# The main expert's two layers as three products of rounded parts, with its raw weights loaded a second time

## The reference

```python
    # attn_out: softmax(q k^T / 8, causal) v, mixed by g with phi(q) M_prev / (phi(q) z_prev)
    x = np.ascontiguousarray(attn_out.transpose(0, 2, 1, 3)).reshape(B * S, H * D)
    # dense part: h = x @ w_in (512 x 2048); g = h, 0 or (h + 1)^2 / 4; x2 = g @ w_out
    logits = x2 @ w_gate
    expert_idx = np.argmax(logits, axis=1)
    # the first 288 tokens of each expert, in order, are kept
    h = np.maximum(np.einsum('ecd,edf->ecf', disp, w1), 0.0)     # 8 x (512 x 1024)
    y = np.einsum('ecf,efd->ecd', h, w2)                         # 8 x (1024 x 512)
    out[i] = gate_w[i] * y[expert_idx[i], pos[i]]                # for kept tokens
```

## Time and profile before

| | |
|---|---|
| median of 3 runs | 315.66 us (315.33 to 315.79) |
| the profiled execution, in all | 316.72 us |
| its span, first to last instruction | 315.0 us |
| mean granted clock of TensorE | 0.999 |
| busy: PE, DVE, ACT, POOL | 307.2, 211.9, 143.5, 122.5 us |

### The profile page before, as it was taken

How to read it: one execution, slowest core, us unless ns; L and a number is a source line. 1 busy time by engine, 2 the same in 40 slices (tenths; PEclk the granted TensorE clock), 3 DMA queues, 4 the chain that set the end, 5 groups by cost and what they waited for, 6 DMA issues and landing times.

```text
span 315.0 us, 6957 instructions
## 1 busy us (share of the span) xinstructions
PE 307.2 (98%) x2697; PEld 249.3 (79%) x2697; DVE 211.9 (67%) x569; ACT 143.5 (46%) x318; POOL 122.5 (39%) x146
## 2 busy tenths in 40 slices
PE   7999999999999999999999999999999999999994
PEld 6566676676677988878999989898989867775764
DVE  4899998999976466987866377657955466612300
ACT  1777865866965144555633353335343322101020
POOL 4777997998998200735860030003000000100121
PEclk9999999999999999999999999999999999999999
DMA  8999986861456600000002229530042075099720
GB/s 158 172 203 213 228 210 104 201 182 34 139 141 143 205 0 2 2 0 2 0 2 37 40 67 401 132 51 1 2 75 40 0 301 235 12 370 402 293 76 10
DMA packets 75047, 38.48 MB, mean 122 GB/s; under 512 B 66008, under 2 KB 66016, under 8 KB 73988
## 3 DMA queue, kind: packets, MB, share of 16 engines
q1 hardware_dynamic: 72340, 36.74, 44.6%
q10 hardware_dynamic: 2416, 0.59, 1.0%
q0 software_dynamic: 256, 0.67, 0.7%
HBM read 32.66 MB, written 5.39 MB: 121 GB/s over the span
## 4 chain that ended last, share of the span: by engine, by line
PE 94%; DVE 3%; issue 1%; POOL 1%; POOLq 0%; DVEq 0%
PE bank_a L1725 17%; PE bank_b L1725 16%; PE bank_out L1682 6%; PE bank_b L1785 4%; PE bank_pt L1785 4%; PE bank_a L1583 4%; PE bank_pt L1635 4%; PE bank_a L1659 3%; PE bank_b L1937 3%; PE bank_a L1937 3%; PE bank_b L1946 3%; PE bank_a L1946 3%; PE bank_b L1578 2%; PE bank_out L1758 2%; PE bank_out L1679 2%; PE bank_out L2074 2%
## 5 line engine op out<-in xcount | busy, mean ns | idle before, releaser
L687 POOL TENSOR_SCALAR prob<-prob,rl,gate_loc 128x512 f32<-128x512 f32 (+3 forms) x64 | 41.7, 665 | 11.8 <-DVE rl L1144 11.8
L1725 PE MATMUL bank_a<-x_hi,win_hi 128*128 128x288 f32 x128 | 39.3, 307 | 0.0
L1725 PE MATMUL bank_b<-x_hi,win_hi 128*128 128x288 f32 x128 | 38.1, 297 | 0.0
L1725 PE MATMUL bank_b<-x_lo,win_hi 128*128 128x288 f32 x128 | 38.0, 297 | 0.0
L1725 PE MATMUL bank_a<-x_lo,win_hi 128*128 128x288 f32 x128 | 38.0, 297 | 0.0
L1725 PE MATMUL bank_b<-x_hi,win_lo 128*128 128x288 f32 x128 | 38.0, 297 | 0.0
L1725 PE MATMUL bank_a<-x_hi,win_lo 128*128 128x288 f32 x128 | 38.0, 297 | 0.0
L923 ACT ACTIVATE g_raw<-bank_a,biases 128x576 f32<-128x576 f32 x16 | 11.9, 743 | 53.3 <-DVE sq L1221 53.3
L860 ACT ACTIVATE prob<-prob,negmax 128x512 f32<-128x512 f32 (+3 forms) x64 | 35.0, 549 | 0.8 <-DVE negmax L1094 0.8
L716 POOL TENSOR_TENSOR x_lo<-xT,x_hi 128x1152 fp32r<-128x1152 f32 x4 | 10.6, 2662 | 63.5 <-ACT x_hi L873 63.5
L1227 DVE TENSOR_TENSOR g_raw<-g_raw,sq 128x576 f32<-128x576 f32 x32 | 31.3, 979 | 0.5 <-ACT sq L924 0.5
(11 more groups left out here) (309 smaller groups left out, 746.6 us busy)
## 6 DMA issues: line engine op xcount, KB each, us to landing
w_sb<-in_moe_w_dram SPq DMA_DIRECT2D x6, 2048.0 KB, 13.9
win_raw<-in_moe_w_in_dram SPq DMA_DIRECT2D x4, 1024.0 KB, 5.8
wout<-in_moe_w_out_dram SPq DMA_DIRECT2D x4, 1024.0 KB, 5.8
win_raw<-in_moe_w_in_dram SPq DMA_DIRECT2D x1, 4096.0 KB, 13.5
out_dram<-zero_row SPq DMA_DIRECT2D x8, 288.0 KB
x_d<-x_rows SPq DMA_DIRECT2D x32, 72.0 KB, 2.1
v_sb<-in_v_dram SPq DMA_DIRECT2D x16, 128.0 KB, 2.6
qn<-in_q_dram SPq DMA_DIRECT2D x24, 72.0 KB, 5.5
```

What stands on the lines that cost most here:

```text
L687: pool.tensor_scalar(prob[u][:, h, :], prob[u][:, h, :], rl[:, c:c + 1], gate_loc[:, 2 * j + h:2 * j + h + 1], ALU.mult, ALU.mult).then_in ...
L1725: last = pe.matmul(h_bank(d)[:, t, :], w[:, m, f:f + P], x[c % 2][:, m, :], start=(m == 0 and n == 0), stop=(m == KT - 1 and n == 2))
```

## The change

- The main expert's layers are made of rounded parts: three products for each fp32 one (`main_first`, `main_second`). `hT` becomes `h_hi` (ACT) and `h_lo` (DVE), `x2T` is split into `x2_hi` (ACT, chunk four, step 5) and `x2_lo` (DVE, chunk four, step 6, before `place`).
- The weights are split while chunks three and four run. ACT rounds w1 in eight blocks (`first_hi`) and w2 in eight (`second_hi`, the last four during the first layer). POOL subtracts the eight of w1 and four of w2, DVE the other four of w2. The lo parts are written over the raw weights in `w1_sb[0]`, `w2_sb[0]`. The hi parts take the places of `xT` and of the x parts.
- Because of that expert 0's raw w1 and w2 are loaded a second time for the left tokens, and the other experts' weights get other places: the first one's is that of `win_hi`, the second one's that of `win_lo`, which is also that of `win_raw`. So w1 of the second waits for `few_hidden` (`s_fh`), and what follows it in SP's list stands behind that wait.
- The second layer runs over f outside and the four outputs inside. `few_x` comes after f = 4, `few_hidden` after f = 5, `few_turned` in the middle of f = 7. `ranks` and `list_tokens` move one tile later.
- The left tokens' experts go in the order 1, 2, 0. Banks are exchanged: the rows' banks become `f_bank[0:3]`, the left tokens' dense part uses `bank_pt` and `bank_o`. `copy_yt` is shared between DVE (0, 1) and ACT (2, 3).

```diff
-        w_at = (w_first_at, xT_at, win_at)
+        w_at = ((w_first_at, w_first_at + 4 * DT * F), (win_at, win_at + 4 * DT * F), (win_lo_at, win_lo_at + 4 * DT * F))
+        w1_hi, _, _ = sb("w1_hi", [P, ET, DM], F32R, at=xT_at)
+        w1_lo, _, _ = sb("w1_lo", [P, DT, F], F32R, at=w_at[0][0])
...
@@ sync
-            expert_weights(0, e0)
+            first_weights(0, e0)
+            second_weights(0, e0)
...
+            sp.wait_ge(s_eh, ET)
+            first_weights(0, e0)
             sp.wait_ge(s_fx, 16)
             sp.wait_ge(s_job, 1)
-            expert_weights(1, sp.value_load(jobs[0:1, 0, 1:2], min_val=0, max_val=E - 1))
-            expert_weights(2, sp.value_load(jobs[0:1, 0, 2:3], min_val=0, max_val=E - 1))
+            others = [sp.value_load(jobs[0:1, 0, k:k + 1], min_val=0, max_val=E - 1) for k in range(1, OTHERS + 1)]
+            first_weights(1, others[0])
+            sp.wait_ge(s_fh, 1)
+            first_weights(2, others[1])
+            second_weights(1, others[0])
+            second_weights(2, others[1])
+            sp.wait_ge(s_ey, DT)
+            second_weights(0, e0)
@@ gpsimd
-            for c in range(2, NCH):
-                x_lo_part(c)
+            x_lo_part(2)
+            for i in range(4):
+                first_lo(i)
+            x_lo_part(3)
+            for i in range(4):
+                second_lo(i)
+            for i in range(4, ET):
+                first_lo(i)
@@ scalar, in chunk(c, first)
+                    if c == 2 and d in (2, 3):
+                        first_hi(2 * d - 4)
+                        first_hi(2 * d - 3)
+                    if c == 3 and d in (0, 1):
+                        second_hi(2 * d)
+                        second_hi(2 * d + 1)
+                    if c == 3 and d in (3, 4):
+                        first_hi(2 * d - 2)
+                        first_hi(2 * d - 1)
+                    if c == 3 and d == 5:
+                        x2_hi_part()
...
+            for f in range(ET):
+                act.wait_ge(s_eh, f + 1)
+                if f == 0:
+                    act.wait_ge(s_g, ND * NCH - 1)
+                act.activation(h_hi[:, f, :], e_bank(f)[:, 0:SLOTS], ACT.Relu).then_inc(s_ehe, 1)
+                if f == 2:
+                    exponentials(NCH)
+                if f in (0, 1, 3, 4):
+                    second_hi((4, 5, 0, 6, 7)[f])
@@ vector
+                    if c == NCH - 1 and d == 6:
+                        x2_lo_part()
                     if c > 0 and d == 6:
                         place(c)
...
             chunks(dve, chunk)
+            hidden_lo(0)
+            hidden_lo(1)
             copy_lt(NCH)
+            hidden_lo(2)
             choose(NCH)
+            second_lo(4)
+            second_lo(5)
+            hidden_lo(3)
             gates_of(NCH)
             place(NCH)
+            hidden_lo(4)
+            hidden_lo(5)
             rank_tokens(NCH)
+            hidden_lo(6)
+            hidden_lo(7)
...
+            second_lo(6)
+            second_lo(7)
             list_jobs()
@@ tensor
+            def main_first(f):
+
+                bank_read(f)
+                pe.wait_ge(s_al, f + 1)
+                if f > 3:
+                    pe.wait_ge(s_ehe, f - 3)
+                    pe.wait_ge(s_hl, f - 3)
+                for m in range(DT):
+                    for n, (w, x) in enumerate(((w1_hi[:, f, m * P:m * P + P], x2_hi), (w1_hi[:, f, m * P:m * P + P], x2_lo),
+                                                (w1_lo[:, m, f * P:f * P + P], x2_hi))):
+                        last = pe.matmul(e_bank(f)[:, 0:SLOTS], w, x[:, m, :], start=(m == 0 and n == 0), stop=(m == DT - 1 and n == 2))
+                last.then_inc(s_eh, 1)
...
+            for f in range(ET):
+                main_first(f)
+                route_between(f)
+            for f in range(ET - 1):
+                main_second(f, range(DT))
+                if f == 4:
                     few_x()
+                if f == 5:
                     few_hidden()
+            main_second(ET - 1, range(2))
+            few_turned()
+            main_second(ET - 1, range(2, DT))
...
-                pe.wait_ge(s_wf[k], 16)
-                pe.wait_ge(s_kte, k + 1)
-                if k == 0:
-                    pe.wait_ge(s_ere, slot_tiles)
+                pe.wait_ge(s_wf[k], 32 if k == 0 else 16)
+                pe.wait_ge(s_kte, ORDER.index(k) + 1)
```

More of the change, by code:

```diff
@@ L241, in build_program @@
         offset[0] = phase
+        y_row = [sb(f"y_row{r}", [ST, DM], F32)[0] for r in range(slot_tiles)]
         x2_few, _, _ = sb("x2_few", [P, DM_PART], F32)
@@ L944, in exponentials, with x2_hi_part, first_hi, second_hi @@
                 act.activation(ex[:, :, :], lg[:, :, :], ACT.Exp).then_inc(s_ex, 1)
+            def x2_hi_part():
+                for n in range(2):
+                    act.wait_ge(s_xst[n], 16 * 4 * NPAIR // 2)
+                act.wait_ge(s_ye, KT)
+                act.activation(x2_hi[:, :, :], x2T[:, :, :], ACT.Copy).then_inc(s_xh, 1)
+            def first_hi(i):
+                if i == 0:
+                    act.wait_ge(s_we[0], 16)
+                    act.wait_ge(s_xre, 4)
+                    act.wait_ge(s_xlo, 2)
+                if i == 4:
+                    act.wait_ge(s_xre, NPAIR)
+                    act.wait_ge(s_xlo, NCH)
+                act.activation(w1_hi[:, i, :].rearrange("p (m c) -> p m c", c=P), w1_sb[0][:, :, i * P:i * P + P], ACT.Copy
+                               ).then_inc(s_ah, 1)
+            def second_hi(i):
+                if i == 0:
+                    act.wait_ge(s_wf[0], 16)
+                    act.wait_ge(s_h, ND * (NCH - 1))
+                if i == 4:
+                    act.wait_ge(s_h, ND * NCH)
+                act.activation(w2_hi[i][:, :], w2_sb[0][:, i, :], ACT.Copy).then_inc(s_bh, 1)
             def chunk(c, first):
@@ L975, in _, with hidden, copy_yt @@
             chunks(act, chunk)
-            def hidden(J, late):
+            def hidden(J):
                 for f in range(ET):
                     act.wait_ge(s_eh, ET * J + f + 1)
-                    if late and f == 0:
-                        act.wait_ge(s_g, ND * NCH - 1)
                     act.activation(hT[:, f, :], e_bank(f)[:, 0:SLOTS], ACT.Relu).then_inc(s_ehe, 1)
-                    if late and f == 2:
-                        exponentials(NCH)
-            hidden(0, True)
+            for f in range(ET):
[7 more added lines that the diff above has]
+                    second_hi((4, 5, 0, 6, 7)[f])
+            def copy_yt(J, m):
+                act.wait_ge(s_ey, DT * J + m + 1)
+                act.activation(yT[:, m, :], e_bank(m)[:, 0:SLOTS], ACT.Copy).then_inc(s_eye, 1)
             act.wait_ge(s_ft, 1)
@@ L1022, in work @@
                     activation_terms(NCH + n, d)
-                hidden(n + 1, False)
+                hidden(n + 1)
             jobs_of(act, work)
@@ L1927, in _, with expert @@
             chunks(pe, chunk)
-            def expert(J, ahead, between, within):
+            def expert(J):
                 for f in range(ET):
-                    ahead(f)
                     if f > 3:
@@ L1947, in expert, with main_second @@
                                          start=(f == 0), stop=(f == ET - 1))
-                        if f == ET - 1:
-                            last.then_inc(s_ey, 1)
-                        within(m, f)
+                    last.then_inc(s_ey, 1)
+            def main_first(f):
[9 more added lines that the diff above has]
+                last.then_inc(s_eh, 1)
+            def main_second(f, outs):
+                pe.wait_ge(s_bl, f + 1)
+                for m in outs:
+                    pe.wait_ge(s_hl, 5 + m if f == 0 else f + 1)
+                    part = slice(m * P, m * P + P)
+                    for n, (w, x) in enumerate(((w2_hi[f][:, part], h_hi), (w2_hi[f][:, part], h_lo), (w2_lo[:, f, part], h_hi))):
+                        last = pe.matmul(e_bank(m)[:, 0:SLOTS], w, x[:, f, :], start=(f == 0 and n == 0), stop=(f == ET - 1 and n == 2))
+                    if f == ET - 1:
+                        last.then_inc(s_ey, 1)
             def expert_rows(J, tiles):
@@ L1998, in few_hidden @@
                 pe.wait_ge(s_fte, 1)
-                pe.wait_ge(s_eye, 1)
+                spread_list()
                 pe.wait_ge(s_win, 16)
@@ L2076, in few_second @@
                                          w2_sb[k][:, f, DM_PART * g:DM_PART * (g + 1)],
-                                         start=(k == 0 and f == 0), stop=(k == OTHERS and f == ET - 1))
-                if k == OTHERS:
+                                         start=(k == ORDER[0] and f == 0), stop=(k == ORDER[-1] and f == ET - 1))
+                if k == ORDER[-1]:
                     last.then_inc(s_ky, 1)
-            for k in range(OTHERS + 1):
+            for k in ORDER:
                 few_first(k)
-            for k in range(OTHERS + 1):
+            for k in ORDER:
```

(4 more changed lines are left out.)

140 lines of the change are left out of this document (84 added, 56 removed).

## The result

| | before | changed |
|---|---|---|
| median | 315.73 us (315.33 to 316.0, 4 runs) | 322.02 us (320.17 to 322.44, 4 runs) |
| the profiled execution, in all | 316.72 us | 322.08 us |
| its span | 315.0 us | 320.3 us |
| mean granted clock of TensorE | 0.999 | 0.987 |

What follows compares the result with a forecast made beforehand. TensorE, 94% of the chain, bounded the kernel. Its 4.2 us gain would become a 4.9 us wait: last landing 309.4 plus 1.8 and 4.4 gives span 315.6, time 316.3 us, range 313.6 to 318.4.

Steps and rivals of the forecast that it cites:

- The products of rounded parts: Main expert's two layers: three products at 0.134 us each replace an fp32 one of 0.51, 6.9 us less TensorE work.
- before `ranks`: End of chunk four: TensorE stands 0.4 us because the new x2_lo delays VectorE's queue.
- before the second logits: End of chunk four: TensorE stands 0.9 us for a later add_terms on VectorE.
- the second layer starts: Main expert's second layer: start at 269.55 against 271.16, a gain of 1.6 of the possible 3.6 us.
- The splits in chunks three and four: Splitting the weights on ScalarE and GpSimd during the hidden layers of these chunks: costed at nothing.
- The gather of x_few and the list of jobs ... are ready before: Ahead of few_hidden: both, made within 5 us of the hot rows, cause no wait; few_hidden ends at 283.6.
- The term of the four loads: Four 2 MB loads issued from 283.7 on, behind few_hidden: 24.2 us plus 1.5 for writes, last landing 309.4.
- The writes of rows: Three writes of finished rows, 0.58 MB, fall amid the four loads: 1.5 us if they queue, 0 if they find gaps.
- C: Last products: TensorE's clock falls while it waits, up to doubling their 1.8 us; time 318.1 us, chance 0.16.
- my own case: End of the kernel: the 4.2 us gain turns into a 4.9 us wait for expert 0's w2; 316.3 us, chance 0.42.
- The base: From span to median: the 0.6 us difference of spans was carried over to the median of 315.66, giving 316.3.
- B: Last products: loads land before TensorE wants them and its 4.2 us gain arrives whole; time 311.5 us, chance 0.12.

Runs made afterwards that it cites:

- e1: The changed kernel without the second load of expert 0's w2, reading the first other expert's w2 instead (output differs): 316.14 us, ratio 1.004.
- e2: The changed kernel without both second loads, expert 0's left products reading the first other expert's weights (output differs): 315.12 us, ratio 1.001.
- e6: The changed kernel with x2_lo made before VectorE's clip of step 6 in chunk four instead of behind it: 320.42 us, ratio 1.0152.
- e8: e7 with x2_lo also made before the clip of step 6 in chunk four: 315.46 us, ratio 1.0002.
- e4: The kernel before with only a second load of the main expert's w1 added, issued 0.7 us after the gather: 315.28 us, ratio 1.0001.
- e3: The changed kernel with w1's second load moved behind the wait for the gather: 320.27 us, ratio 1.0153.
- e5: The changed kernel with 28 unused transposes after each of the first two thirds of the last products: 320.91 us, ratio 1.0181.
- e10: The changed kernel run once more, as it is: 321.22 us, ratio 1.0168.
- e7: The changed kernel without second loads: expert 0 first, from its hi and lo parts, and the first other's w2 loaded before the few_hidden wait: 317.0 us, ratio 1.0047.
- e9: e8 with expert 0's w1 loaded again behind the gather and the first other's w2 back behind few_hidden: 315.29 us, ratio 0.9995.
- e11: e9 with 64 more small instructions at TensorE's start (10 whole and 72 small transposes for 18 whole): 316.69 us, ratio 0.9994.
- e14: e9 with 16 more small instructions at TensorE's start (10 whole and 24 small transposes for 18 whole): 315.77 us, one run.
- e16: e9's program once more, beside e15 on the same chip: 315.31 us, ratio 0.9938.
- e13: The changed kernel with 64 more small instructions at TensorE's start: 323.51 us, ratio 1.02.
- e15: e9 with 56 more small instructions at TensorE's start (4 whole and 70 small transposes for 18 whole): 315.09 us, ratio 0.9939.
- e12: e9 with SyncE's wait for few_hidden moved to the end of the w_out products, keeping queues empty there: 321.31 us, one run.

## Why the prediction came out as it did

**Right, by its own steps.** The products of rounded parts are 0.13 apart, 12 in 1.57 to 1.77 us, as costed. `x2_lo` takes 1.35 us. TensorE stands before `ranks` (0.15 against 0.4) and before the second logits (1.02 against 0.9). The whole trace is some 0.4 us late, already at the load of w1 at 186.26 (185.87 before), ahead of every new instruction of the change; the traces of the other runs that start like it have this load at 185.4 to 186.5, so it is scatter. Apart from that the second layer starts at 269.7 (270.06 - 0.4) against 269.55. The splits in chunks three and four cost nothing: the load behind chunk four, at 252.86 against 252.47, is late by the same 0.4. The loads became last, and TensorE's gain became a wait: e1 and e2 show it by taking loads away, and e6 against e8 by making the same edit once with the loads last and once without.

**The step that failed first: "The gather of x_few and the list of jobs ... are ready before".** I listed the second load of w1 as lying "under the second layer" and did not ask what it does to the small transfer behind it. The gather took 6.71 us, landing at 278.8, and TensorE waited for it. SyncE's list stood as long, so w1 of the first other was issued at 280.1 and not at 277. `few_hidden` ended at 285.0, where 283.6 + 0.4 was forecast: 1.0 us. The wait itself is 0.61 of it. e4 shows that a load beside the gather stretches it, and e3, without that load ahead, that `few_hidden` then ends 0.8 us earlier. The end gained less than that in e3, since its load of w1 then stood among the bytes behind the gather. So of the late end this step is the smaller part, and the queue of loads the larger.

**The term of the four loads was mis-sized.** Forecast were 24.2 + 1.5 = 25.7 us from the first issue to the last landing, measured 27.3 (285.15 to 312.42). Ahead of the four the queues still held w1 of the first other, issued late, which landed at 287.6. I had drawn the 24.2 from a stretch in which nothing went before. The writes of rows took 6.6 us to land (3.6 in e4), so they did meet full queues; what they cost the loads of the 1.5 us, no row separates. The full queues moved 381 to 415 GB/s in the stretches shown, against the 435 that the prediction cites from the Trainium skill, "DMA: Bandwidth & Descriptors", section Specifications.

**The clock was not a rival but a companion.** I gave C a chance of 0.16 beside my own case, though my own case already held a wait of 4.9 us. After waits of 3.0 and 2.7 us the granted clock was 0.50, and the last 64 products took 3.28 us, 1.5 more than the 1.8 of the sum; e5 shows that it is the clock. I should have put both in one case. By the Trainium skill, "TensorE: Matmul & The Clock Gate", section What's actually happening, the throttled state is the default and activity releases it. The traces agree: 0.50 after the waits, and 1.00 in e5, where transposes fill them.

**The base.** I carried the difference of spans over to the median. But before's profiled execution was 1.1 us above its own median (316.72 and 315.66), and the changed one's was not (322.08 and 322.02). The sum of the misses: 0.4 + 1.0 + 1.6 + 1.5, with 0.1 for the tail, is 4.6 of the 4.7 us between the spans (320.3 and 315.6), and 1.0 to 1.1 from the base gives the 5.7 us between 316.3 and 322.0. This is read from one trace; e10's has the last load 1.1 us later.

**Slips that changed nothing.** The second layer's saving is 16.3 - 12.8 = 3.5 us, not 3.3, and the sum did not use it. 283.6 + 2.8 + 0.45 + 0.9 is 287.75, not 287.85. And the "over 500 GB/s" against B holds only with the 4 us of start and tail taken off: 8.4 MB between 283.7 and 304.5 are some 400 GB/s.

**Not foreseen: the stops.** In the changed kernel itself they cost nothing, since the wait behind them shrinks by as much. In the traces of the variants where TensorE sets the end (e7 to e9, e11, e14 to e16) all stops together took 0.8 to 2.7 us, and with them a good part of the 4.2 us that the products of parts had brought.

## What to carry to other kernels

Price a load that moves behind a later wait as a queue: all bytes still ahead of it at the measured rate, and ask of each new big load which small transfer comes right behind it. If the sum ends in a wait of several us ahead of dense TensorE work, price that work at the lower clock in the same case. It is not certain: 64 products took 1.96 us after a wait of 3.13 us in e13, and 3.64 us after one of 3.32 us in e3. And splitting weights in place is not free when the raw values are needed later: keeping both parts costs TensorE twice the small products of that expert (some 3.5 us, by 32 in 1.73 and 64 in about 1.8), but saves 4 MB of loads, and came out at 1.0047 (e7) where loading again had 1.0168 and 1.0189. With `x2_lo` early it was 1.0002 (e8) against 1.0152 (e6).

## What the runs showed of the hardware that I had not expected

- A gather of 64 KB took 2.7 to 3.2 us to land on quiet queues, and 5.6 to 6.8 us with a 2 MB load issued from 2.2 us ahead of it to 0.7 us behind it.
- The profile has a DMA queue of the kind "instruction" with packets of 0.02 MB. With the other queues full TensorE stopped for 0.4 to 2.1 us, and each of these stops ended 1.8 to 2.9 us after such a packet had passed. The first stop moved one for one with 16 instructions more ahead of it, and was gone with 56 or 64 more or with the queues empty (e14, e15, e11, e12). That the packets are TensorE's list is the reading that fits.
- 64 column-tiled products take 1.95 us at a granted clock of 1.00 and 3.64 us at 0.50 (e5, e6). A stop alone can bring the lower level: behind e6's, of 2.02 us, the granted clock was 0.50 from 294 to 296, and eight turns took 1.84 us in place of 1.08.
- The kernel before differed by 0.5 to 0.7% between chips (315.2 to 315.4 against 317.0 and 317.3 us), while e9's program did not (315.29 and 315.31 us, two chips).
